# Sparse expert layer: the next tile's rows are turned inside the up-projection, and the upper block of the expert rows inside the second down block

## The reference

```python
def _moe2_ref(x, expert_emb, tau, w1, w2):
    ...
    expert_idx = np.argmax(logits, axis=1)
    ...
    gate_w = probs[np.arange(N), expert_idx]
    for e in range(E):
        mask = expert_idx == e
        if not mask.any():
            continue
        h = np.maximum(x[mask] @ w1[e], 0.0)
        out[mask] = gate_w[mask, None] * (h @ w2[e])
    return out
```

## Time and profile before

| | us |
|---|---|
| median of 3 executions | 1569.25 (1569.08 to 1570.49) |
| the profiled execution, its device time | 1569.61 |
| the profiled execution, span of its instructions | 1567.6 |
| PE busy in the span | 1546.3 (99%) |
| DVE / ACT / POOL busy | 686.0 / 516.5 / 338.1 |

### The profile page before, as it was taken

The page is one execution under the profiler, slowest core; times in us unless marked ns, Lnnn a source line. Parts: engine busy times, 40 slices in busy tenths (PEclk is TensorE's granted clock), DMA queues, the critical chain, the costliest instruction groups (busy, mean ns, idle before and its releaser), DMA issues.

```text
span 1567.6 us, 21713 instructions
## 1 busy us (share of the span) xinstructions
PE 1546.3 (99%) x7513; PEld 1293.7 (83%) x7514; DVE 686.0 (44%) x1242; ACT 516.5 (33%) x946; POOL 338.1 (22%) x563
## 2 busy tenths in 40 slices
PE   8999999999999999999999999999999999999997
PEld 7999997888888888888888888888888887788886
DVE  7999995433222211211322131131232255887665
ACT  6888885012111100101211110111121133676554
POOL 4565656000300300120030030012004000243222
PEclk9999999999999999999999999999999999999999
DMA  6545561101100100110110011011002121774310
GB/s 159 138 114 144 127 179 55 54 1 54 55 1 0 72 36 0 54 54 0 42 65 0 0 58 49 0 54 54 0 26 81 41 81 75 248 263 163 119 40 25
DMA packets 44776, 108.88 MB, mean 69 GB/s; under 512 B 5783, under 2 KB 7831, under 8 KB 44737
## 3 DMA queue, kind: packets, MB, share of 16 engines
q1 hardware_dynamic: 41088, 99.83, 20.3%
q0 software_dynamic: 3424, 8.14, 1.6%
q10 hardware_dynamic: 224, 0.39, 0.1%
HBM read 81.57 MB, written 8.13 MB: 57 GB/s over the span
## 4 chain that ended last, share of the span: by engine, by line
PE 96%; DVE 2%; ACT 1%; issue 1%; POOL 0%; DVEq 0%; POOLq 0%; ACTq 0%
PE psum L478 27%; PE psum L479 26%; PE psum L480 26%; PE psum L786 4%; PE psum L773 2%; PE psum L800 2%; PE psum L799 2%; PE psum L774 2%; PE psum L1119 1%; PE psum L754 1%; PE psum L813 1%; PE psum L920 1%; PE psum L1110 0%; DVE pt_lo L1437 0%; ACT prob L1175 0%
## 5 line engine op out<-in xcount | busy, mean ns | idle before, releaser
L1308 ACT ACTIVATE h_hi<-psum 128x512 fp32r<-128x512 f32 x192 | 114.9, 598 | 878.5 <-PE psum L480 878.5
L478 PE MATMUL psum<-w_lo,h_hi 128*128 128x512 f32 x768 | 304.3, 396 | 0.0
L479 PE MATMUL psum<-w_hi,h_hi 128*128 128x512 f32 x768 | 302.4, 394 | 0.0
L478 PE MATMUL psum<-xt_lo,w_hi 128*128 128x512 f32 x768 | 300.3, 391 | 0.0
L480 PE MATMUL psum<-xt_hi,w_lo 128*128 128x512 f32 x768 | 298.9, 389 | 0.0
L479 PE MATMUL psum<-xt_hi,w_hi 128*128 128x512 f32 x768 | 298.9, 389 | 0.0
L480 PE MATMUL psum<-w_hi,h_lo 128*128 128x512 f32 x768 | 298.5, 389 | 0.0
L1743 DVE SCALAR_TENSOR_TENSOR h_lo<-psum,h_hi 128x512 fp32r<-128x512 f32 x192 | 133.0, 693 | 351.4 <-ACT h_hi L1308 351.4
L509 POOL CAST w_hi<-w_raw 128x512 fp32r<-128x512 f32 x68 | 41.7, 613 | 801.4 <-PE psum L480 801.0
L1806 DVE SCALAR_TENSOR_TENSOR tok<-psum,route,tok 128x512 f32<-128x512 f32 x83 | 56.8, 745 | 358.5 <-PE psum L480 358.5
L480 PEld LDWEIGHTS psum<-w_hi,h_lo 128*128 128x128 f32 x768 | 144.2, 188 | 32.5
(11 more groups left out here) (272 smaller groups left out, 2004.9 us busy)
## 6 DMA issues: line engine op xcount, KB each, us to landing
w_raw<-in_moe_w_dram SPq DMA_DIRECT2D x25, 2048.0 KB, 8.2
w_raw_odd<-in_moe_w_dram SPq DMA_DIRECT2D x4, 2048.0 KB, 10.6
k_hh<-k_hi SPq DMA_DIRECT2D x32, 192.0 KB, 3.0
w_raw_even<-in_moe_w_dram SPq DMA_DIRECT2D x3, 2048.0 KB
x_rows<-tok SPq DMA_DIRECT2D x14, 256.0 KB, 2.4
k_raw<-in_k_dram SPq DMA_DIRECT2D x8, 384.0 KB, 3.2
v_raw<-in_v_dram SPq DMA_DIRECT2D x16, 192.0 KB, 3.5
q_b<-q_hi SPq DMA_DIRECT2D x16, 192.0 KB, 4.0
```

Source lines behind the costliest of these rows:

```text
L478: pe.matmul(acc, a[0], b[1], start=start, stop=False)
L479: pe.matmul(acc, a[0], b[0], start=False, stop=False)
L1308: act.activation(h_s[0][:, f, :], psum[:, f % 4, :], ACT.Relu).then_inc(m1.h_hi, 1)
```

## The change

The diff, whole:

```diff
-    def matmul_x3(pe, acc, a, b, start, stop):
+    def matmul_x3(pe, acc, a, b, start, stop, inside=None):
 
         pe.matmul(acc, a[0], b[1], start=start, stop=False)
         pe.matmul(acc, a[0], b[0], start=False, stop=False)
+        if inside is not None:
+            inside()
         return pe.matmul(acc, a[1], b[0], start=False, stop=stop)
...
                         if c == 1 and kd == 2:
                             turn_h(i, 0)
+                            turn_row(i + 1)
                         mm = matmul_x3(pe, psum[:, c, :], [x[:, kd, :] for x in x_s],
                                        [w[:, kd, c * 512:(c + 1) * 512] for w in w1_s], kd == 0, kd == KD - 1)
                     mm.then_inc(s_up2, 1)
-                turn_row(i + 1)
                 pe.wait_ge(m2.w2_lo, KF * (i + 1) if more else KF * (first + 1))
                 pe.wait_ge(s_y2, i + 1)
                 for f in range(KF):
                     if f % 4 == 0:
                         pe.wait_ge(s_g_lo, 2 * i + f // 4 + 3)
-                    if f == 1:
-                        turn_h(i, 1)
                     mm = matmul_x3(pe, psum[:, 4, :], [g[:, f, :] for g in g_s], [w[f] for w in w2_p[u]],
-                                   f == 0, f == KF - 1)
+                                   f == 0, f == KF - 1, inside=(lambda: turn_h(i, 1)) if f == 1 else None)
                 mm.then_inc(s_down2, 1)
...
                     if c == 0:
                         if more:
                             w2_hi2(e + 1, 1 - u, w2_raw_of[1 - u], (KF - 1,))
+                        act.wait_ge(s_up2, 2 * i + 2)
                         x_hi(i + 1)
```

## The result

The changed kernel takes 1574.89 us (median of 7 executions, 1573.62 to 1576.24), the kernel before 1569.39 us (7 executions in the same sessions). The ratio is 1.0033, with a 95% interval of 1.0023 to 1.0042: slower by 5.5 us. The profiled execution took 1574.72 us.

What follows compares the result with a forecast made beforehand. The prediction took the kernel as PE-bound with DVE just behind; 9 x 0.25 plus 7 x 0.44 plus under 0.05 gave 5.4 us, so 1574.7 us against the 1569.25 median, range 1571.0 to 1577.0.

Steps and rivals of the forecast that it cites:

- `f` = 4 in the inner tiles: Load waiting for `g_lo` starts at U (last up-projection matmul's start) + 3.58, 0.36 late; 0.25 us lost in 9 tiles.
- the step on prices: On PE, a waiting load costs 0.11 to 0.12 us less than its lateness; each `x_row` transpose costs 0.11 us.
- The change of expert: DVE's `w1_lo` keeps its distance from U, which comes 0.44 us later; 0.44 us lost at each of 7.
- Expert 7's tile: No next expert's weights to split on DVE; the `f` = 4 load 0.15 late, costing under 0.05 us.
- The run of eight transposes: On PE, eight in a row expose eight loads as two times four do: cost 0.
- The upper `turn_h`: Moved back two matmuls, which repay what `turn_row` no longer covers ahead of its slot: cost 0.
- The added wait on ACT: `x_hi` now waits for the end of the up-projection, the same moment to 0.01 us: cost 0.
- The gather: `turn_row` needs `x_row` about 1.4 us sooner, but a gather lands within 6.3 us of a 12.35 us tile: cost 0.
- That eight transposes pack closer: Rival: the merged run on PE saves 0.2 us per tile, 2.1 us slower in all, 1571.4; chance 0.05.
- That `f` = 4 does not bind: Rival: DVE runs faster and the `f` = 4 load does not wait; down to 1567.4, at most no change; chance 0.10.
- That only `f` = 4 counts: Rival: changes of expert recover, leaving 0.25 in 16 tiles, 4.0 us, 1573.2; chance 0.07.
- That the stalls add up: Rival: 0.36 lost whole in 16 tiles plus 0.44 at changes of expert, 8.9 us, 1578.1; chance 0.05.

Runs made afterwards that it cites:

- e6: Changed kernel with the last `w1_lo` piece at the 7 changes of expert cut to 8 of 1024 columns: 1573.07 us, ratio 1.0024.
- e4: Changed kernel with its run of eight transposes cut in two, `turn_row` placed ahead of kd = 3: 1575.08 us, ratio 1.0034.
- e1: Kernel before with only the `x_row` transposes moved into the up-projection, upper `turn_h` left whole ahead of `f` = 1: 1575.51 us, ratio 1.0041.
- e2: Kernel before with only the upper `turn_h` moved, inside the product `f` = 1, `turn_row` left behind the up-projection: 1572.72 us, ratio 1.0020.
- e3: Changed kernel with two of the four `x_row` transposes inside the up-projection and two behind it: 1572.84 us, ratio 1.0021.
- e5: Changed kernel with `w2_lo` piece 5 moved ahead of the relu of block 1 on DVE, PE's order unchanged: 1572.59 us, ratio 1.0019.
- e7: Kernel before with the last `w1_lo` piece at the 7 changes of expert cut to 8 of 1024 columns: 1568.64 us, ratio 0.9997.

## Why the prediction was right

**The sum.** 5.4 us were predicted over the profiled execution of before, 5.5 were measured, and the stretch of tiles grew by 5.44. The terms, from the timelines:

- *`f` = 4 in the inner tiles*: 0.25 us predicted, 12.35 to 12.60 measured in nine tiles. The load was to start at U + 3.58 and did, in 0.02 us. It came 0.36 us late and the tile lost 0.25, so a late load costs 0.11 less than its delay, as the step on prices had it.
- *The change of expert*: 0.44 predicted, 12.50 to 12.93 measured. U to the waiting load was to stay at 8.72 and is 8.71. That the stall at `f` = 4 of such a tile is inside the 0.44 is shown by e6: take the 0.44 away, and the 0.25 appears.
- *Expert 7's tile*: its load was to come 0.15 late, at U + 3.37, and comes at U + 3.38. No lower `turn_h` follows, so its price of under 0.05 is in no distance.
- *`f` = 0*: the sum has no term for the first wait on `g_lo`, and the prediction gives no reason for leaving it out. Before, `turn_row` stood ahead of it and its load at U + 0.56, 0.12 to 0.22 us after the lower `g_lo`. Now the load is held by that `g_lo` in every tile and starts at U + 0.03 to 0.06, where U + 0.00 would be its slot. That is within the 0.11 us that costs nothing. In the first tiles of experts 0, 1, 3 and 5 it is 0.12 to 0.37 late, and the idle time ahead of `f` = 4, which hangs on U, takes it up. The term is 0 as it turned out, but that was luck: the prediction did not look at it.
- *The run of eight transposes*: 0 predicted. 0.44 from the first run to the second (1466.86 to 1467.29 is 0.43) and 0.44 to the real start of the next matmul (1467.29 to 1467.73). e4 shows it by the time too.
- *The upper `turn_h`*: 0 predicted. It starts at U + 1.40, where it was U + 1.37 (only in the first two tiles is it later, U + 1.65 and U + 1.52), and e1 shows what it costs if it isn't moved: 0.31 us in a tile.
- *The added wait on ACT*: 0 predicted. `x_hi` starts at U + 0.51 and not at U + 0.43, 0.08 later than I had it, and `x_lo` does not wait for it. Removing that wait alone was not tried, since `x_hi` would then overwrite rows that the last up matmuls still read.
- *The gather*: 0 predicted; no wait of PE for `x_row` is in the list.

**The rivals.** That eight transposes pack closer falls by the rows above; and a smaller price for each transpose would have held for the two runs of four as well, so that it was no reason to expect a gain from merging them. That `f` = 4 does not bind falls by its 17 waits. That only `f` = 4 counts falls by the 12.93 us. That the stalls add up falls by e6.

**Where sizes were off.** The expectations of e2, e3 and e5 were 0.5, 0.9 and 1.4 us too low, and that of e1 1.2 too high. About half of the last is that an inner tile of e1 loses 0.31 and not 0.37; the span of its profiled execution is 6.1 us over before, not 5.6, and the rest is inside its interval. Of what e2, e3 and e5 cost more, two parts are seen. The inner tiles of e2, e3 and e5 lose 0.06 to 0.08 where 0.03 to 0.06 were worked out. And the first tiles of experts 3 and 5 are 12.59 to 12.64 us long in these three kernels, 0.17 to 0.22 more than the inner tiles around them; in the changed kernel they are 12.60, like the rest. Expert 1's tile, too, is 0.09 to 0.13 longer than the other last tiles. What is late in these tiles shows at the start of expert 3 in e3:

```profile
1383.31 4.62 DVE L1730 TENSOR_TENSOR w_lo<-w_raw_odd,w_hi 128x1024 fp32r<-128x1024 f32 x4
...
1388.12 1.29 DVE L1736 TENSOR_TENSOR xt_lo<-w_raw_even,xt_hi 128x512 fp32r<-128x512 f32 x2 [0.18 <-issue]
...
1390.07 0.47 PEld L1123 LDWEIGHTS psum<-ident,g_row 128*128 128x128 f32 x4 [0.16 <-DVE g_row L1871]
...
1391.74 0.68 DVE L1875 TENSOR_TENSOR g_lo<-psum,g_hi 128x512 fp32r<-128x512 f32 x1
...
1392.53 0.19 PEld L478 LDWEIGHTS psum<-w_lo,g_hi 128*128 128x128 f32 x1 [0.18 <-issue]
```

DVE idles 0.18 us with nothing to wait for, where its loop over pairs of experts turns (ahead of experts 3 and 5; 0.11 us where it is entered, ahead of expert 1). In these tiles the lower `turn_h` stands right behind DVE, and so does `f` = 0: U is 1391.99, its load starts 0.11 us after the lower `g_lo`, at U + 0.54, and in the inner tiles it stands at U + 0.34. The 0.20 go on to the upper `turn_h` (U + 1.82, not 1.62), to `g_hi`, `g_lo` and `f` = 4 (U + 3.82, not 3.62), since here these hang on PE and not on DVE's queue. That is the length of the tile. At the other changes of expert DVE goes on at once.

For the loop's turn as the cause speak e6 and e7. Behind their shortened `w1_lo` DVE idles 0.96 to 1.06 us at these three places and 0.38 to 0.56 at the other changes. At the other changes it waits for ACT: ahead of expert 4 in e7 ACT's first piece of `w2` ends at 1410.67 and DVE starts at 1410.69. Ahead of expert 3 the view names ACT too, but its piece ends at 1385.82 and DVE starts at 1386.43. So the turn takes DVE about 1 us, which a whole last piece of `w1_lo` (1.22 us) mostly hides. This is argued from the rows; a kernel without the turn was not tried. Why 0.18 us stick out ahead of experts 3 and 5 in e2, e3 and e5 and none in the changed kernel and in that of before, at the same turn, stays open.

What is left of the differences, some 0.5 us in e5, is no more than the half width of its interval.

Two differences between the profiled executions are not the change's. Before the first tile's `turn_h` the profiled execution of before ran PE at a granted clock of 0.71 on average (1346.0 to 1351.8 us), part of it (0.50 from 1346.2 to 1349.0 us) at the 1.2 GHz level, and that of the changed kernel at 1.00, the 2.4 GHz level. From the first up matmul to that `turn_h` it took 5.76 us before and 4.84 after, and the layer began 0.73 us later (1346.04 and 1346.77). Nothing ahead of the layer was changed. The two nearly cancel, which is why the spans differ by no more than the stretch of tiles. PE, earlier there than DVE, then waits 0.5 us for the relu, and the first tile took 13.06 us and not 12.93. Of the nine profiles only that of e3 also shows 1.00 in this stretch, and its first tile took 13.05 us and not 12.76. Without that 0.13 us the stretch grew by 5.3, and the terms for its 16 tiles add up to the same.

No version beats the kernel before by anything that can be measured. With the waits at the changes of expert gone (e7), the stretch of tiles is 0.65 us shorter, and no wait of PE for DVE is long enough for the list.

## What to carry to other kernels

On an engine that is always busy, moving a piece of work may cost nothing by itself, as here (e4); what counts is which event it is moved across. Write down the moment on which the next engine's queue hangs, here the end of the up-projection, and measure every wait from it: work moved ahead of it makes that queue late by its whole length, and the slack of each wait behind it shrinks by as much. Do this for every wait, the ones that look safe too: the first wait on `g_lo` was left out here, and its slack, 0.1 us or less, was gone as well. A wait that passes by 0.1 us shows in no list of waits, so look for it in the timeline before moving anything past it; and if filler work on the late engine can go into the idle time that the move opens, as in e5, part of the loss comes back.

## What the runs showed of the hardware

A weight load of 0.19 us in the profile holds up its matmul by only 0.11 where it had to wait, if the start of the load behind it is taken for the matmul's real start: 1472.46 to 1472.57 in the changed kernel, the same as in the earlier trace rows. The sum of idle loads therefore overstates the price: 6.0 us idle on `g_lo` in the 17 tiles of e6, of which 4.0 stand in its distance from e7 (the seventeenth, 0.21 idle, lies behind that distance).

From the end of a DVE instruction to the start of the load that waits for it, the rows show 0.05 to 0.06 us at `f` = 4 (1472.40 to 1472.46) and 0.11 to 0.12 us at `f` = 0 (1468.80 to 1468.92). At `f` = 0 the program waits for two more semaphores just before; whether these make the difference was not tried.
